# A two-layer network in float32r pieces: layer 2 ten units behind layer 1, relu and square ahead of the logarithm, a reordered prologue, outputs stored by halves

## Reference

```python
w = softmax(weight)                                   # (8 heads, 7 taps)
out = np.einsum('hk,bskhg->bshg', w, x_unf)           # x_unf: the 7 last tokens
# layer 1
h = x @ w_in
P = a[0] + a[1] * h + a[2] * h2 + a[3] * h3
Q = 1.0 + np.abs(b[0]) * np.abs(h) + np.abs(b[1]) * h2
x = (P / (Q + 1e-06)) @ w_out
# layer 2
r = np.maximum(x @ w_in2, 0.0)
return (s * (r * r) + b) @ w_out2
```

## Time and profile before

| | |
|---|---|
| median of three runs | 1307.58 us |
| profiled execution, its own time | 1309.7 us |
| span of the profiled execution | 1307.9 us |
| mean granted TensorE clock | 0.991 |
| TensorE busy | 1276.3 us (98%) |
| VectorE busy | 1138.5 us (87%) |
| ScalarE busy | 1115.1 us (85%) |
| GpSimd busy | 331.7 us (25%) |

### The profile page before, as it was taken

How to read it: one execution, slowest core, us unless ns; L and a number is a source line. 1 busy time by engine, 2 the same in 40 slices (tenths; PEclk the granted TensorE clock), 3 DMA queues, 4 the chain that set the end, 5 groups by cost and what they waited for, 6 DMA issues and landing times.

```text
span 1307.9 us, 16349 instructions
## 1 busy us (share of the span) xinstructions
PE 1276.3 (98%) x5984; PEld 1077.7 (82%) x5984; DVE 1138.5 (87%) x1048; ACT 1115.1 (85%) x1072; POOL 331.7 (25%) x147
## 2 busy tenths in 40 slices
PE   5897999999999999999999999999999999999998
PEld 3665888888888888888888888888888888888887
DVE  5998889998999989998899989999899998979830
ACT  5887898888889888889888888998888898888843
POOL 4333222222222222222222222222222222222210
PEclk8998999999999999999999999999999999999999
DMA  5211000010000100001000010001000000000000
GB/s 137 106 33 25 1 1 13 1 37 1 12 0 0 36 0 12 0 0 36 0 12 0 13 23 0 12 0 36 0 12 0 0 12 1 13 1 13 1 13 13
DMA packets 14045, 20.40 MB, mean 16 GB/s; under 512 B 1472, under 2 KB 9664, under 8 KB 13504
## 3 DMA queue, kind: packets, MB, share of 16 engines
q1 hardware_dynamic: 13872, 20.00, 5.4%
q10 hardware_dynamic: 144, 0.01, 0.0%
HBM read 13.72 MB, written 6.29 MB: 15 GB/s over the span
## 4 chain that ended last, share of the span: by engine, by line
PE 90%; DVE 5%; ACT 2%; issue 2%; POOL 1%; DMA 0%; DVEq 0%; SPq 0%; ACTq 0%
PE o L363 25%; PE h L337 9%; PE h L338 9%; PE h L340 9%; PE h L341 9%; PE h L339 9%; PE o_tail L352 4%; PE o L350 4%; PE o_tail L354 4%; PE o L351 4%; PE o L353 4%; DVE work L737 1%; DVE work L704 1%; DVE work L706 1%; DVE work L739 1%
## 5 line engine op out<-in xcount | busy, mean ns | idle before, releaser
L320 POOL TENSOR_TENSOR gl<-work,gh 128x1024 fp32r<-128x1024 f32 x128 | 307.0, 2398 | 896.2 <-ACT gh L566 896.2
L363 PE MATMUL o<-v,work 128*128 128x192 f32 x2048 | 353.3, 326 | 0.0
L363 PEld LDWEIGHTS o<-v,work 128*128 128x128 f32 x2048 | 339.2, 190 | 10.1
L704 DVE SCALAR_TENSOR_TENSOR work<-work,coef,h 128x1024 f32<-128x1024 f32 x128 | 163.7, 1279 | 91.9 <-ACT work L539 91.9
L337 PE MATMUL h<-x_hi,w_hi 128*128 128x512 f32 x512 | 224.4, 438 | 17.6 <-DVE work L709 13.4
L341 PE MATMUL h<-x_tail,w_tail_lo 128*128 128x512 f32 x512 | 205.0, 400 | 0.0
L338 PE MATMUL h<-x_lo,w_hi 128*128 128x512 f32 x512 | 204.6, 400 | 0.0
L340 PE MATMUL h<-x_tail,w_tail_hi 128*128 128x512 f32 x512 | 204.6, 400 | 0.0
L339 PE MATMUL h<-x_hi,w_lo 128*128 128x512 f32 x512 | 204.2, 399 | 0.0
L537 ACT ACTIVATE work<-h,coef 128x1024 f32<-128x1024 f32 x128 | 154.2, 1205 | 27.8 <-PE h L341 21.4
L569 ACT ACTIVATE work<-work 128x1024 f32<-128x1024 f32 x128 | 135.7, 1060 | 42.4 <-DVE work L704 38.8
(11 more groups left out here) (78 smaller groups left out, 1544.8 us busy)
## 6 DMA issues: line engine op xcount, KB each, us to landing
out_dram<-y_out SPq DMA_DIRECT2D x16, 384.0 KB, 2.6
xt<-in_x_main_dram SPq DMA_DIRECT2D x7, 518.0 KB, 4.5
xt_tail<-in_x_tail_dram SPq DMA_DIRECT2D x8, 259.0 KB, 5.1
work<-in_moe_w_out_dram SPq DMA_DIRECT2D x1, 1536.0 KB, 9.7
v<-in_moe_w_out_dram SPq DMA_DIRECT2D x1, 1536.0 KB, 6.3
work<-in_moe_w_in_dram SPq DMA_DIRECT2D x1, 1024.0 KB, 8.4
work<-in_moe_w_in_dram SPq DMA_DIRECT2D x2, 512.0 KB, 5.8
xt<-in_x_main_dram SPq DMA_DIRECT2D x2, 259.0 KB, 6.4
```

What stands on the lines that cost most here:

```text
L320: nc.gpsimd.tensor_tensor(gl[:, j % 2, :], r_buf[j % 2], gh[:, j % 2, :].bitcast(F32), ALU.subtract).then_inc(gl_ready, 1)
L363: last = pe.matmul(o2[:, c // 2, c % 2, 0:D], g, v2[:, f, :], start=(f == 0 and c % 2 == 0), stop=(f == FT - 1), skip_group_check=True)
L704: nc.vector.scalar_tensor_tensor(q_buf[buf], w_abs, b0_abs, h_flat, ALU.add, ALU.mult).then_inc(z_done, 1)
```

## The change

1. **Distances.** SKEW 11 to 10, OUT1_LAG 3 to 2, X2_STEP stays 2 and Y_STEP becomes 2 (it was 3). The split of `o1` moves ahead of L704's step in its unit, and GpSimd waits for it before that unit's `gl`.
2. **TensorE's order in a unit** becomes: first product of layer 1, second product of layer 2, first product of layer 2, second product of layer 1. The second product of layer 1 waits for `gh` alone, runs its six matmuls on `gh`, then waits for `gl`. Layer 2's first unit of a tile waits for `x2` part by part.
3. **ScalarE's order in a unit** of the loop becomes t, w, `gh`, absolute, relu, square, logarithm, exponential, and the logarithm goes into `r_buf`. For units 1 to 10 t and w are made ahead, between the previous unit's absolute and logarithm (unit 1's before unit 0's absolute, in buffers of their own), and for units 0 to 7 `gh` is made one unit earlier, between logarithm and exponential.
4. **Prologue.** TensorE takes 5 taps of the first convolution in place of 4, VectorE 2 in place of 3, and TensorE does 3 taps of the second convolution before the first unit. The load of the second x moves ahead of w_out1; piece 1 of w1 is rounded before unit 0; VectorE's split of v1 waits until GpSimd has made w1's first low parts; w1's last piece is made in halves. w2 is loaded and split in halves and quarters, spread over units 2 to 13, and the tail's diagonals get a place of their own and are made at units 5 to 7.
5. **Output** is stored by two DMAs of half the size, and the last second product of a tile finishes one half of `o2` before the other.

The diff, cut:

```diff
-    SKEW = 11
-    OUT1_LAG = 3
+    SKEW = 10
+    OUT1_LAG = 2
-    X2_STEP = OUT1_LAG - 1
+    X2_STEP = OUT1_LAG
...
-    TAPS_AT = {(0, 1): (("pair", 0), ("tail", 0)), (0, 4): (("pair", 1),), (0, 5): (("pair", 2), ("tail", 1)),
-               (0, 6): (("pair", 3), ("tail", 2)), (0, 7): (("pair", 4), ("tail", 3)),
-               (1, 0): (("pair", 5), ("tail", 4)), (1, 1): (("pair", 6), ("tail", 5)), (1, 4): (("tail", 6),)}
+    TAPS_AT = {(0, 3): (("pair", 0), ("tail", 0)), (0, 4): (("pair", 1), ("tail", 1)), (0, 5): (("pair", 2), ("tail", 2)),
+               (0, 6): (("pair", 3), ("tail", 3)), (0, 7): (("pair", 4), ("tail", 4)),
+               (1, 0): (("pair", 5), ("tail", 5)), (1, 3): (("pair", 6), ("tail", 6))}
-    PE_TAPS_OF_FIRST = (3, 4, 5, 6)
-    DVE_TAPS_OF_FIRST = (0, 1, 2)
+    PE_TAPS_OF_FIRST = (2, 3, 4, 5, 6)
+    DVE_TAPS_OF_FIRST = (0, 1)
+    TAPS_BEFORE_UNITS = (0, 1, 2)
...
+        W2_HIGH_AT = {2: ("tail", 0), 4: ("main", 0), 5: ("main", 1), 11: ("tail", 1)}
+        W2_LOW_AT = {4: ("tail", 0, 0), 5: ("tail", 0, 1), 6: ("main", 0, 0), 7: ("main", 0, 1),
+                     8: ("main", 1, 0), 9: ("main", 1, 1), 12: ("tail", 1, 0), 13: ("tail", 1, 1)}
...
+                    if j == X2_STEP and tile(t - 1):
+                        pool.wait_ge(x2_tail_lo_ready, counted(t))
...
+            pe.wait_ge(diag_ready, TAPS)
+            pe.wait_ge(x0_second_loaded, 16)
+            conv_taps(1, xt[:, 1, :], TAPS_BEFORE_UNITS, 0, TAPS - 1)
...
+            def second_product_1(n, k, buf):
+                pe.wait_ge(gh_ready, counted(n - OUT1_LAG + 1))
+                for half in range(2):
...
+                pe.wait_ge(gl_ready, counted(n - OUT1_LAG + 1))
+                for half in range(2):
...
-                    if unit(n - OUT1_LAG):
...
-                        pe.wait_ge(gh_ready, counted(n - OUT1_LAG + 1))
-                        pe.wait_ge(gl_ready, counted(n - OUT1_LAG + 1))
-                        second_product_1(k, (j - OUT1_LAG) % 2)
                     if tile(t):
                         second_product_of_layer_2(t, j, m, k2)
...
+                    if unit(n - OUT1_LAG):
+                        second_product_of_layer_1(n, j, t)
...
+            def first_steps(n, h_flat, t_of_n, w_of_n):
+                act.wait_ge(h1_ready, counted(n + 1))
+                nc.scalar.activation(t_of_n, h_flat, ACT.Identity, bias=a2, scale=a3).then_inc(t_ready, 1)
+                nc.scalar.activation(w_of_n, h_flat, ACT.Abs, scale=b1_abs).then_inc(w_ready, 1)
...
+                    if ahead(n + 1) and n > 0:
+                        act.wait_ge(t3_done, 1 if n == 1 else n + 1)
+                        first_steps(n + 1, h2_flat if in_h2(n + 1) else h1_flat, t_buf, w_abs)
+                    if unit(n):
+                        act.wait_ge(q_ready, counted(n + 1))
+                        act.wait_ge(gl_ready, counted(n - 1))
+                        nc.scalar.activation(r_buf[buf], q_buf[buf], ACT.Ln, bias=one_eps).then_inc(ln_done, 1)
+                    if cast_early(n - 1):
+                        high_of_g(n - 1, 1 - buf)
...
+            dve.wait_ge(w_lo_ready, 4)
             low_of_weight(v1_lo[:, :, :], raw_v1[:, :, 0:P], v1_hi[:, :, :], 3)
...
+                    if j == X2_STEP and tile(t - 1):
+                        split_o1(t, hi, lo)
+                        sum_o1_tail(t)
+                        split_o1_tail(t, tail)
```

More of the change, by code:

```diff
@@ new lines, in second_product_1, with first_product_of_layer_2 @@
+                last.then_inc(out1_done, 1)
+            def first_product_of_layer_2(k, x2p, t2):
+                c = [slice((2 * k + half) * P, (2 * k + half + 1) * P) for half in range(2)]
+                if k == 0:
+                    pe.wait_ge(x2_hi_ready, counted(t2 + 1))
+                for half in range(2):
+                    pe.matmul(h2[:, half, :], w2_hi[:, c[half]], x2_hi[x2p][:, :], start=True, stop=False)
+                    pe.matmul(h2[:, half, :], w2_lo[:, c[half]], x2_hi[x2p][:, :], start=False, stop=False)
+                if k == 0:
+                    pe.wait_ge(x2_lo_ready, counted(t2 + 1))
+                for half in range(2):
+                    pe.matmul(h2[:, half, :], w2_hi[:, c[half]], x2_lo[x2p][:, :], start=False, stop=False)
+                if k == 0:
+                    pe.wait_ge(x2_tail_hi_ready, counted(t2 + 1))
+                    pe.wait_ge(x2_tail_lo_ready, counted(t2 + 1))
+                for half in range(2):
+                    pe.matmul(h2[:, half, :], w2_tail_hi[:, c[half]], x2_tail[x2p][:, :], start=False, stop=False)
+                    last = pe.matmul(h2[:, half, :], w2_tail_lo[:, c[half]], x2_tail[x2p][:, :], start=False, stop=True)
+                last.then_inc(h2_ready, 1)
@@ new lines, in second_product_2, with product @@
+            def second_product_2(k, buf):
+                def product(half, c):
+                    f = 2 * k + half
+                    g = g2[buf][:, half * TOK + c * P:half * TOK + (c + 1) * P]
+                    return pe.matmul(o2[:, c // 2, c % 2, 0:D], g, v2[:, f, :],
+                                     start=(f == 0 and c % 2 == 0), stop=(f == FT - 1), skip_group_check=True)
+                if k == UNITS - 1:
+                    for bank in range(2):
+                        for half in range(2):
+                            for c in (2 * bank, 2 * bank + 1):
+                                last = product(half, c)
+                        if bank == 0:
+                            last.then_inc(out2_half_done, 1)
+                else:
+                    for half in range(2):
+                        for c in range(SUB):
+                            last = product(half, c)
@@ L366, in second_product_2, with conv_taps @@
                 last.then_inc(out2_done, 1)
-            def conv_taps(bank, rows, taps, first, last):
+            def conv_taps(bank, rows, taps, first, last, diagonals=diag):
                 for k in taps:
-                    done = pe.matmul(conv_bank[bank], diag[k], rows[:, k:k + TOK], start=(k == first),
+                    done = pe.matmul(conv_bank[bank], diagonals[k], rows[:, k:k + TOK], start=(k == first),
                                      stop=(k == last))
@@ L438, in phase @@
                     early = isinstance(n, int) and n < SKEW
-                    if unit(n) and not early:
+                    if unit(n) and not (isinstance(n, int) and n <= SKEW):
                         product_of_layer_1(n, j, t, parity)
@@ new lines, in phase @@
+                    if second(t) and j == 2:
+                        act.wait_ge(conv_summed, 5)
+                        copy_of_conv(conv_tail[:, :], 1)
+                    if isinstance(n, int) and n in W2_HIGH_AT:
+                        rows, half = W2_HIGH_AT[n]
+                        if rows == "main":
+                            act.wait_ge(w2_loaded[half], 16)
+                            high_of_weight(w2_hi[:, W2_HALF[half]], raw_w2[half])
+                        else:
+                            act.wait_ge(w2t_loaded[half], 32)
+                            high_of_weight(w2_tail_hi[:, W2_HALF[half]], raw_w2_tail[half])
```

270 lines of the change are left out of this document (146 added, 124 removed).

## The result

The changed kernel takes **1292.93 us** (median of 4 runs, 1292.05 to 1294.03) against 1308.48 for the kernel before on the same chip (4 runs, 1306.75 to 1309.45): ratio 0.9883, 95% interval [0.9866, 0.9900]. The forecast was 1290.6. The profiled execution took 1294.03, with a span of 1292.2 where before's was 1307.9: 15.7 us less, where 17.0 were forecast.

The account below looks back on a forecast made before the run. TensorE bounds the loop, VectorE the start. Unit 11's start at 104.5 + 1179.7 + 1.0 + 1.0 + 1.3 = 1287.5, with 3.4 behind it a span of 1290.9; forecast median 1290.6, 8-in-10 range 1284.5 to 1300.5.

Parts of the forecast that it names:

- Behind the last matmul: After TensorE's end: half of L715 runs earlier and the last store is half as big, leaving 3.4 of 4.2 us.
- z(0): Start of VectorE's L704 of unit 0: 22.6, 1.9 earlier; bounds 21.7 and 23.9, the latter at the lower clock.
- z(1): Start of VectorE's L704 of unit 1: 26.4, where it was 32.68.
- settling: At units 11 and 12, w and so `gl` late behind ScalarE's copies, half a us twice: 1.0.
- the longer units at x2: Loop units where x2's split makes VectorE late for TensorE: 0.07 more for each of 14 tiles, 1.0.
- the drain's wait: At the end TensorE waits about 1.3 for GpSimd's last `gl`, no longer hidden by a third unit of lag.
- the 1.9 taken off for matmuls at the lower clock: From unit 11 on, 1.9 less work than before for ten matmuls at the lower clock.
- Unit 10: TensorE waits some 2.5 us for x2, then runs at the lower clock, adding 1.3; unit 11 starts at 104.5.
- Head stays TensorE's: Rival, 13%: lower clock returns in units 2 to 9, 1.9 per spell of 3.5 us; 1296 to 1300.
- x2 a stall: Rival, 12%: x2, L715 and a late L704 meet; TensorE stands 0.8 us a tile, not 0.3: 1298.
- the wait of every unit: Slower rival, 6%: TensorE waits for `gl` in each unit past a margin of 0.5; 1325 at 0.3 a unit.
- Two signs that I had named for being wrong: In the loop: units exceeding 9.6 us, or a wait for `gl` showing.

Follow-up runs that it names:

- unit 1 in turn: The changed kernel with ScalarE making t and w of unit 1 behind unit 0's exponential again: 1296.71 us, ratio 0.9913 to the kernel before.
- one edit: The changed kernel with layer 1's second product waiting for `gh` and `gl` together at its first matmul: 1421.39 us, ratio 1.0862 to the kernel before.

## Why the prediction came out right

**Where the 15.7 us come from.** Unit 12's first product starts 9.6 earlier (114.77, and 124.38 in the earlier trace rows). Layer 2 is one unit further by then, and what TensorE still has to do is shorter by that unit: 1174.4 in place of 1179.3, 4.9 less. Behind the last matmul it is 3.06 in place of 4.21. That is 9.6 + 4.9 + 1.2. The forecast had the first two in its head; the loop had only to stay as it was, and its experiments show what keeps it so. What the smaller pieces of w2, the spread diagonals and the halved stores bring one by one no run separates.

**The head** came by the steps: z(0) by VectorE's split of v1 behind GpSimd's pieces (18.97, forecast 18.6), z(0) to z(1) by VectorE's own 3.73 and 0.23 of waiting for ScalarE (3.96 where 3.8 was forecast; undoing the order costs 3.2 here and 3.8 in all), then six intervals of 7.42 with the bias row (7.74) and x1's split (9.76) between them, and x1's split no longer blocked (L752 0.42 at 60.11, where the 2.29 of the earlier trace rows stood). That z(0) fell on the number is luck in part, two errors that cancel: the split started 0.4 late, since the sum came at 14.62 and not 14.1, and it took 3.56 and not 3.96, since its second pass, clear of GpSimd, took 1.22. The first product without the taps would have cost 1.2 more and not 2.3, and z(0) then does follow it.

**The rule on the first matmuls.** The Trainium skill (TensorE: Matmul & The Clock Gate, "What's actually happening") says that the count of matmuls at the low clock differs from run to run. By that z(0) could have been 23.9. For the first product no trace here bears it out: with the taps ahead of it the granted clock was 1.00 in the changed kernel's trace and in all the others. At unit 10 the traces agree with it: equal rests, with the spell and without.

**From 105.19 on.** The sum had 1183.0 to TensorE's end (1179.7 + 1.0 + 1.0 + 1.3) and it was 1184.0 (1289.15 - 105.19). By its terms: settling cost 0.1 and not 1.0 (units 11 to 13 take 9.58 and 9.71); the longer units at x2, against each kernel's own ordinary unit, went from 3.1 to 4.1, the 1.0 forecast; the drain's wait was about 1.0, not 1.3. That leaves 2.1 unforeseen, hidden in part by the 1.1 that these terms had too much. About 1.5 of it is a hundredth of a us per unit: 86 ordinary distances are 9.586 in the mean, where before 86 had 9.573. With SKEW 12 they are 9.584, so it is not the distance; what it is no run here tells, and it stays open. Some 0.3 is the 1.9 taken off for matmuls at the lower clock: unit 12 of the kernel before took 11.21, 1.6 over. Behind the last matmul it took 3.1, forecast 3.4.

**Unit 10.** The term was right in size and I took it as sure: I put the lower clock at 1.3, what lasts of it is 1.1, and it comes in some executions only. Unit 11's start, 0.7 later than forecast, holds 2.3 for it, of which 0.85 comes back since the wait for ScalarE's copy would have cost that anyway.

**The rivals.** *Head stays TensorE's:* one of its spells did come, behind the 2.27 ahead of unit 2; after that TensorE rested only 0.64 and 0.75 up to unit 10. VectorE hid it: L835's intervals are 7.42 outside the splits (7.74 with the bias row), and GpSimd's pieces did not slip. With unit 1 in turn the spell was twice as long and VectorE had to wait 1.1 for TensorE, so this rival was nearer than the intervals of 7.42 show. *x2 a stall:* 14 waits of at most 0.4 as before. `gl` *the wait of every unit:* it did not come in the change, but one edit brings it (+128). My margin of 0.5 for it was right: `gl` ends 0.4 to 0.5 ahead of the matmul that reads it in 85 of 113 units of the loop, and never less than 0.05. Two signs that I had named for being wrong do show, both small: a wait for `gl` in the loop (3.3 us of weight loads in 8 units) and units over 9.6 (the longer ones, 9.68 to 9.88); the ordinary unit is 9.59. Where I was wrong is in costing ScalarE's new order at nothing either way. It isn't slack: the order before, with the new lag and the logarithm in `r_buf`, costs 51 us, which neither the sum nor a rival held, because I had counted ScalarE's place in the row but not the buffer its logarithm writes.

**VectorE beside GpSimd.** The Trainium skill (SBUF — State Buffer, "Who interferes with whom") says that a VectorE instruction with two inputs in SBUF contends with a GpSimd one that reads it. The traces agree, in both directions: VectorE's pass takes 3.40 beside a `gl`, 1.23 alone, and GpSimd's piece 2.83 beside the split when nothing holds that back, 0.74 alone.
